# A fused attention and feed-forward kernel: the range check moves to GpSimd, the decayed state to VectorE

## What is computed

```python
for t in range(S):                       # attention, per batch and head
    cur = einsum('bhd,bhe->bhde', u * k_t, v_t)
    y[t] = einsum('bhd,bhde->bhe', r_t, state + cur)
    state = w_t[..., None] * state + einsum('bhd,bhe->bhde', k_t, v_t)
h = x @ w_in;  solu = h * softmax(h);  x = layernorm(solu, g_ln) @ w_out   # expert 1
h = x @ w_in2; x = maximum(0.01 * h, h) @ w_out2                           # expert 2
```

## Time and profile before

| | |
|---|---|
| median of three runs | 825.48 us (825.39 to 825.62) |
| profiled execution: its own time | 825.48 us |
| profiled execution: span | 823.7 us |
| TensorE matmul (PE) busy | 786.2 us, 95% |
| VectorE (DVE) busy | 521.3 us, 63% |
| ScalarE (ACT) busy | 338.8 us, 41% |
| GpSimd (POOL) busy | 196.7 us, 24% |
| mean granted TensorE clock | 0.978 |

### The profile page before, as it was taken

One profiled execution on the slowest core, in us unless ns is written; L12 is line 12 of the kernel. 1 busy time (PEld: TensorE's weight loads), 2 busy tenths in 40 slices (PEclk: granted clock), 3 DMA queues, 4 the chain that ended last, 5 costly groups with the idle time before them and its releaser, 6 DMA issues.

```text
span 823.7 us, 11957 instructions
## 1 busy us (share of the span) xinstructions
PE 786.2 (95%) x4570; PEld 746.2 (91%) x4570; DVE 521.3 (63%) x1068; ACT 338.8 (41%) x652; POOL 196.7 (24%) x216
## 2 busy tenths in 40 slices
PE   2877999999999999999999999999999999999996
PEld 2655999999999999999999999999999999999996
DVE  7778776576575676667665765666765775553332
ACT  3335644344433444434434444335443444334332
POOL 4477823113111221121221131122131121000000
PEclk9976899999999999999999999999999999999999
DMA  7772211203202302203202122113112030000000
GB/s 193 248 228 58 58 30 29 58 2 87 58 1 58 87 1 58 58 1 88 58 1 58 28 61 58 29 29 87 29 30 58 1 87 30 1 1 29 1 0 32
DMA packets 18847, 43.50 MB, mean 53 GB/s; under 512 B 2272, under 2 KB 14688, under 8 KB 18400
## 3 DMA queue, kind: packets, MB, share of 16 engines
q1 hardware_dynamic: 14736, 33.24, 16.5%
q10 hardware_dynamic: 4048, 9.44, 3.3%
HBM read 37.95 MB, written 4.72 MB: 52 GB/s over the span
## 4 chain that ended last, share of the span: by engine, by line
PE 85%; DVE 0%; ACT 0%; issue 0%; ACTq 0%
PE BANKS L964 60%; PE MISC L964 21%; PE BANKS L1075 2%; PE MISC L994 1%; PE MISC L987 1%; DVE Rraw L863 0%; DVE RL L869 0%; ACT RH L633 0%; ACT Rraw L626 0%; DVE X2L L875 0%; ACT X2H L638 0%; ACT OUT L644 0%; DVE A L745 0%; DVE nmean L817 0%; ACTq L248 0%
## 5 line engine op out<-in xcount | busy, mean ns | idle before, releaser
L626 ACT ACTIVATE Rraw<-BANKS 128x384 f32<-128x384 f32 x128 | 62.9, 492 | 239.5 <-PE BANKS L964 237.8
L863 DVE TENSOR_TENSOR Rraw<-BANKS,Rraw 128x384 f32<-128x384 f32 x128 | 71.3, 557 | 133.5 <-ACT Rraw L626 133.0
L964 PE MATMUL BANKS<-RH,W4H 128*128 128x384 f32 x384 | 138.6, 361 | 0.9 <-DVE RL L869 0.8
L964 PE MATMUL BANKS<-X2H,W3H 128*128 128x384 f32 x384 | 130.4, 339 | 0.2 <-DVE X2L L875 0.2
L964 PE MATMUL BANKS<-X2L,W3H 128*128 128x384 f32 x384 | 129.1, 336 | 0.0
L964 PE MATMUL BANKS<-RL,W4H 128*128 128x384 f32 x384 | 129.1, 336 | 0.0
L964 PE MATMUL BANKS<-X2H,W3L 128*128 128x384 f32 x384 | 129.0, 336 | 0.0
L964 PE MATMUL BANKS<-RH,W4L 128*128 128x384 f32 x384 | 129.0, 336 | 0.0
L633 ACT ACTIVATE RH<-Rraw 128x384 fp32r<-128x384 f32 x128 | 67.1, 524 | 73.2 <-DVE Rraw L863 73.2
L436 POOL TENSOR_TENSOR ke<-att 112x512 f32<-112x512 f32 x24 | 29.5, 1230 | 255.3 <-DVE att L739 255.3
L735 DVE RECIPROCAL ki<-att 112x128 f32<-112x128 f32 x96 | 90.1, 941 | 0.0
(11 more groups left out here) (117 smaller groups left out, 1509.3 us busy)
## 6 DMA issues: line engine op xcount, KB each, us to landing
att<-rkw SPq DMA_DIRECT2D x48, 288.0 KB, 4.9
rtok<-r_tok SPq DMA_DIRECT2D x24, 192.0 KB, 4.5
ktok<-k_tok SPq DMA_DIRECT2D x24, 192.0 KB, 4.6
vtok<-v_tok SPq DMA_DIRECT2D x24, 192.0 KB, 4.7
out<-OUT SPq DMA_DIRECT2D x8, 576.0 KB, 5.6
W3raw<-w_in ACTq DMA_DIRECT2D x1, 3072.0 KB, 11.2
W4raw<-w_out ACTq DMA_DIRECT2D x1, 3072.0 KB, 24.3
W1raw<-w_in ACTq DMA_DIRECT2D x1, 1536.0 KB, 9.5
```

The costliest lines, as they stand in the source:

```text
L626: nc.scalar.activation(Rraw[:, fp % 2, :], PR[fp % 2][:, 0:ST], ACT.Copy, scale=0.01).then_inc(act_slope, 1)
L863: nc.vector.tensor_tensor(Rraw[:, fp % 2, :], PR[fp % 2][:, 0:ST], Rraw[:, fp % 2, :], ALU.max).then_inc(dve_relu, 1)
L964: return nc.tensor.matmul(dst, lhsT, rhs, start=start, stop=stop, skip_group_check=True)
```

## The change

Three things change. The reciprocals are written into `ke` itself, so `ki` and `junk` go, and `inverse` waits for the transposes of the previous chunk's `ke` in place of the range sums. The range check becomes one sum: `end_keys` on GpSimd first adds `ke` (the reciprocals) and `ct` into a spare place (`range_of`: a part of `LN` for the first three chunks, `A` for the others), then makes the end keys, and ScalarE sums that place in one pass in slot 1 of the chunk. The mask of pair 0 waits for this pass where `A` is the place. And `decayed_state` goes from GpSimd: VectorE writes the masked new part into `fresh`, waits for it, and forms the state in four instructions, one per pair.

```diff
+        def range_of(b, m):
+            place = LN[:, CPS - 1, 0:PAIRS * CH] if first(b, m) else A[:, :, :, :].rearrange("p a h t -> p (a h t)")
+            return place[0:PD, :].rearrange("p (a t) -> p a t", a=PAIRS)
             def end_keys(b, m):
                 wait(pool, dve_keys, chunks(b, m, 1, 1))
-                wait(pool, pe_keT, chunks(b, m))
+                if first(b, m):
+                    wait(pool, act_range, m)
+                else:
+                    wait(pool, pe_y, chunks(b, m, PAIRS))
+                nc.gpsimd.tensor_tensor(range_of(b, m), ke[:, :, :], ct[:, p, :, :], ALU.add).then_inc(pool_range, 1)
+                wait(pool, pool_range, chunks(b, m, 1, 1))
                 nc.gpsimd.tensor_tensor(ke[:, :, :], kt[:, p, :, :], last, ALU.mult).then_inc(pool_ke, 1)
-            def decayed_state(b, m):
-                wait(pool, dve_state, states(b, m - 1))
-                nc.gpsimd.tensor_tensor(fresh[:, :, :], state[:, :, :], last, ALU.mult).then_inc(pool_decay, 1)
...
-                        if 0 < m % CPB < CPB - 1:
-                            decayed_state(b, m)
...
-            def take_range(b, m):
-                wait(act, dve_inv, chunks(b, m, PAIRS, PAIRS))
-                for i, part in enumerate((ki[:, :, :], ct[:, m % 2, :, :])):
-                    wait(act, act_range, chunks(b, m, 2, i))
-                    nc.scalar.activation(junk[:, :, :], part, ACT.Copy,
-                                         accum_out=spread[:, bass.ds(chunks(b, m, 2, i), 1)]).then_inc(act_range, 1)
...
             def item_end(b, m, s, attend=True):
-                if attend and s == 7 and exists(b, m) and exists(b, m + 1):
-                    take_range(b, m + 1)
+                if attend and s == 1 and exists(b, m):
+                    wait(act, pool_range, chunks(b, m, 1, 1))
+                    nc.scalar.activation(range_of(b, m), range_of(b, m), ACT.Copy,
+                                         accum_out=spread[:, bass.ds(at, 1)]).then_inc(act_range, 1)
...
             def inverse(b, m, a):
                 if a == 0:
-                    wait(dve, act_range, chunks(b, m, 2))
+                    wait(dve, pe_keT, chunks(b, m))
                 wait(dve, dve_decay, chunks(b, m, PAIRS, a + 1))
-                nc.vector.reciprocal(ki[:, a, :], ct[:, m % 2, a, :]).then_inc(dve_inv, 1)
+                nc.vector.reciprocal(ke[:, a, :], ct[:, m % 2, a, :]).then_inc(dve_inv, 1)
...
             def mask(b, m, a):
+                if a == 0 and not first(b, m):
+                    wait(dve, act_range, chunks(b, m, 1, 1))
...
             def take_state(b, m):
-                    wait(dve, pool_decay, fresh_count(b, m))
-                    for h in range(2):
-                        cols = slice(h * D, (h + 1) * D)
-                        ins = nc.vector.scalar_tensor_tensor(
-                            state[:, :, cols], own[:, :, cols], heads[:, h * D:h * D + 1], fresh[:, :, cols],
-                            ALU.mult, ALU.add)
+                    nc.vector.tensor_tensor(fresh[:, :, :], own, which, ALU.mult).then_inc(dve_fresh, 1)
+                    wait(dve, dve_fresh, fresh_count(b, m))
+                    for a in range(PAIRS):
+                        ins = nc.vector.scalar_tensor_tensor(
+                            state[:, a, :], state[:, a, :], ct[:, m % 2, a, CH - 1:CH], fresh[:, a, :],
+                            ALU.mult, ALU.add)
```

More of the change, by code:

```diff
@@ L134, in build @@
         ke = sb("ke", [PD, PAIRS, CH])
-        ki = sb("ki", [PD, PAIRS, CH])
-        junk = sb("junk", [PD, PAIRS, CH])
         rb = sb("rb", [PD, PAIRS, 2, CH])
@@ L162, in build @@
         mhalf = sb("mhalf", [CH, 1])
-        spread = sb("spread", [PD, 2 * NCH])
+        spread = sb("spread", [PD, NCH])
         total = sb("total", [PD, 1])
@@ L215, in build @@
         dve_decay, dve_inv, dve_keys, dve_masked = sem("dve_decay"), sem("dve_inv"), sem("dve_keys"), sem("dve_masked")
-        dve_diag, dve_y, dve_state = sem("dve_diag"), sem("dve_y"), sem("dve_state")
+        dve_diag, dve_y, dve_fresh, dve_state = sem("dve_diag"), sem("dve_y"), sem("dve_fresh"), sem("dve_state")
         dve_x, dve_max, dve_nmax, dve_he = sem("dve_x"), sem("dve_max"), sem("dve_nmax"), sem("dve_he")
@@ L221, in build @@
             sem("pool_q"), sem("pool_ke"), sem("pool_ruk"), sem("pool_dv"), sem("pool_rstd"), sem("pool_bias"))
-        act_range, pool_decay = sem("act_range"), sem("pool_decay")
+        pool_range, act_range = sem("pool_range"), sem("act_range")
         judged, pe_tame, guarded = sem("judged"), sem("pe_tame"), sem("guarded")
@@ L433, in end_keys @@
                 wait(pool, dve_keys, chunks(b, m, 1, 1))
-                wait(pool, pe_keT, chunks(b, m))
+                if first(b, m):
[4 more added lines that the diff above has]
+                wait(pool, pool_range, chunks(b, m, 1, 1))
                 last = ct[:, p, :, CH - 1:CH].broadcast_to([PD, PAIRS, CH])
                 nc.gpsimd.tensor_tensor(ke[:, :, :], kt[:, p, :, :], last, ALU.mult).then_inc(pool_ke, 1)
-            def decayed_state(b, m):
-                wait(pool, dve_state, states(b, m - 1))
-                last = ct[:, m % 2, :, CH - 1:CH].broadcast_to([PD, PAIRS, PC])
-                nc.gpsimd.tensor_tensor(fresh[:, :, :], state[:, :, :], last, ALU.mult).then_inc(pool_decay, 1)
             def own_token(b, m, part):
@@ L614, in item_end @@
             def item_end(b, m, s, attend=True):
-                if attend and s == 7 and exists(b, m) and exists(b, m + 1):
-                    take_range(b, m + 1)
+                if attend and s == 1 and exists(b, m):
+                    at = chunks(b, m)
+                    wait(act, pool_range, chunks(b, m, 1, 1))
+                    nc.scalar.activation(range_of(b, m), range_of(b, m), ACT.Copy,
+                                         accum_out=spread[:, bass.ds(at, 1)]).then_inc(act_range, 1)
                 for n in due(b, m, s, "rows"):
@@ L673, in _ @@
             part_heads(0, 0)
-            take_range(0, 0)
             for i in range(1, LEAD + 1):
@@ L732, in inverse @@
                 if a == 0:
-                    wait(dve, act_range, chunks(b, m, 2))
+                    wait(dve, pe_keT, chunks(b, m))
                 wait(dve, dve_decay, chunks(b, m, PAIRS, a + 1))
-                nc.vector.reciprocal(ki[:, a, :], ct[:, m % 2, a, :]).then_inc(dve_inv, 1)
+                nc.vector.reciprocal(ke[:, a, :], ct[:, m % 2, a, :]).then_inc(dve_inv, 1)
             def undecayed_keys(b, m):
                 wait(dve, dve_inv, chunks(b, m, PAIRS, PAIRS))
-                nc.vector.tensor_tensor(kt[:, m % 2, :, :], kt[:, m % 2, :, :], ki[:, :, :],
+                nc.vector.tensor_tensor(kt[:, m % 2, :, :], kt[:, m % 2, :, :], ke[:, :, :],
                                         ALU.mult).then_inc(dve_keys, 1)
@@ L915, in _ @@
             run(B - 1, batch_steps(True))
-            dve.wait_ge(act_range, 2 * NCH)
+            dve.wait_ge(act_range, NCH)
             nc.vector.tensor_reduce(total[:, :], spread[:, :], AX.X, ALU.add).then_inc(judged, 1)
```

## The result

The changed kernel takes 835.62 us (median of four, 833.29 to 835.84) against 825.55 of the kernel before (four, with one more than above): a ratio of 1.0113, 95% interval 1.0094 to 1.0133. It is slower, as forecast, but by 10.1 us and not by 2.3, and outside the range. The profiled execution took 836.03 us (span 834.3), against 825.48 (823.7).

What follows compares the result with a forecast made beforehand. TensorE was taken as the bound, full from 105 us on, with losses only in the start. (a) to (d) gave 2.0 us at 80 us; with (e), (f) and the clock, +2.3: 827.8 us, range 826.2 to 829.4.

Steps and rivals of the forecast that it cites:

- the steady part at 0: After the start: slack hides the later end keys and state, so 0 us, with 0 to 1 for the range.
- The price of the state update, +0.7 us: VectorE, each of 16 chunks: product and four short instructions cost 0.7 us more than the L771 pair (0.3 to 1.35).
- The work by engine: Whole kernel: ScalarE 19 us less work, VectorE 11 us more, GpSimd 10 to 14 us more.
- (a): Second chunk's scans, from 13.3 us: GpSimd's extra addition holds the fourth scan too, delaying mask and token loads by 0.8 us.
- (b): Third chunk's values and scans, to 57 us: 0.7 of the 0.8 us is carried there (0.3 to 0.9).
- (c): Third chunk, L781 at 66.72 us: the state before it is 0.7 us longer, so +0.2 (0 to 0.9).
- (d): Fourth chunk, from 69.3 us: GpSimd's addition goes in front of L436 in a chain without cover, +1.1 us.
- (e): Fourth chunk, L781 at 92.65 us: the longer state costs +0.6, or 0 if TensorE's clock makes it late.
- (f): Fifth chunk, L436 at 98.98 us: addition costs 1.0, GpSimd is 0.6 us earlier, so +0.4 (0 to 1.0).
- The clock, -1.0 to +0.9: Start: -1.0 us if the clock still rises at 90.5 us; rising with the work or later, 2.0 to 2.9 in all.
- one turn worse: Rival, 1%: a further 3 us at half clock cost 1.5 us, giving 829.3 us.
- the rivals: Delay absorbed in the start (27%, 826.4 us), VectorE binding the steady part (7%, 833), faster (5%, 823.7), clock worse (1%, 829.3).

Runs made afterwards that it cites:

- e3_state_psum: The changed kernel with the masked new part written back into its PSUM bank, so the four short instructions read one SBUF operand: 828.64 us.
- e2_range_only: The changed kernel with the state part undone (GpSimd decays the state again, two instructions L771); the new range check stays: 829.32 us.
- the fillers in the changed kernel: The changed kernel with unread 128x128 products on TensorE behind the transposes of y in the third and fourth chunk: 834.71 us.
- e6_add_behind: e3_state_psum with the reciprocals in a tile of their own again and GpSimd's range-check addition behind the end keys: 827.38 us.
- the kernel before with fillers: The kernel before with unread 128x512 products on TensorE ahead of the third and fourth chunk's first products with the values: 826.91 us.

## Why the prediction was wrong, point by point

**What bounds the kernel; the steady part at 0.** Right. TensorE is as full as before, its waits are 1.5 us, and the state part from the fifth chunk on measures as nothing.

**The price of the state update, +0.7 us.** Right where nothing holds it: in e3_state_psum the four take 0.99 us (0.85 assumed), with 0.56 for the product, so 1.6 against 0.74, +0.8. The estimate that the prediction worked out from the Trainium skill's "VectorE: DVE Perf Modes" (the section on the TRN2 errata) was 0.16 us for one short instruction. The trace doesn't agree: it has 0.31, and 0.25 for each of four in a row.

**The work by engine.** ScalarE has 18.8 us less over the whole span (19 forecast), VectorE 16.7 more (11) and GpSimd 18.9 more (10 to 14). GpSimd's surplus comes from the additions, 1.5 us each on average where 1.05 to 1.23 was taken, and some 5.5 us of VectorE's is the hold of the state update.

**(a) +0.8.** The mechanism was right, with the size somewhat off: 1.3 us at the scans (4.57 for 3.28). The new addition takes 1.26 us and not 1.05, and GpSimd starts its run 0.35 us later (13.64 for 13.29), because the first scan does. An addition there alone is +0.9 at the end, with the reserve said above.

**(b) 0.7 carried to the third chunk.** 1.5 us. It is the 1.4 us of (a) at the mask (18.38 for 17.01) carried on, of which 0.35 was already there at the first scan (8.19 after, 7.84 before), which waits for its load.

**(c) +0.2 for the state ahead of `XL` in the third chunk.** This step failed. It took the 0.7 us of an undisturbed update minus 0.42 of slack, and put the hold by GpSimd's split at nothing. Product and four instructions take 3.4 us where L771 took 0.74. TensorE lost 2.4 us from 57 to 71 us, and the chunk alone costs 3.3 at the end.

**(d) +1.1.** Right, with 1.3 measured: from the end of GpSimd's one-column instruction to that of `ke` it is 80.12 - 77.51 = 2.6 us, against 74.92 - 73.64 = 1.3. Moving the addition behind gives 1.3 us back in this chain, and 0.9 at the end, which the intervals neither confirm nor exclude.

**(e) 0 to +0.6 in the fourth chunk.** This failed for the same reason, and it is the largest miss: 4.0 us between the transposes of y and the first product with W1, and 5.4 at the end for the chunk alone.

**(f) +0.4.** Not seen in the changed kernel: with TensorE so late, `ke` of the fifth chunk (from 104.33 on) is there long before it is wanted (110.51). The key product did come through sooner, as the step says (1.16 us in place of 3.13). In e2_range_only, where TensorE is earlier, it was held for 6.87, and TensorE did wait for `ke`.

**The clock, -1.0 to +0.9.** The low clock lasted longer, 44 us of the start for 34, as in the rival "one turn worse". TensorE loses 2.1 us between the fourth chunk's first product with W1 and the fifth chunk's transposes, where its products run at half clock to 107 us (0.63 us each for 512 columns, 0.40 after). What the clock costs by itself stays open: the fillers in the changed kernel met a longer hold.

What was missing in (c) and (e) was in the prediction's own rows. Step (a) read from the earlier trace rows that a scan, with both operands in SBUF, waits for GpSimd's instruction to end. The diff gives the state update the same kind of operands, and puts it beside splits of 2.35 us. The key product of the kernel before (3.13 us for 0.68 at 92.56) is a plainer row of the same kind, and wasn't used. I priced it by the size of its data and by L771, which reads PSUM. The Trainium skill has the rule in "SBUF — State Buffer", in the section on SBUF's two separate sides: VectorE with two SBUF inputs and a GpSimd instruction that reads SBUF share a pair of ports, and whichever starts first keeps it for its whole instruction. The trace agrees with it three times: 2.13 and 2.42 us behind splits of 2.35, 1.15 us for a scan behind one of GpSimd's products of about 1 us, and 0.99 for four once an operand comes from PSUM.

None of the rivals named it either: they put the cost into the steady part, the clock or nowhere.

No version here beats the kernel before. The nearest with both parts of the change is e6_add_behind, at +1.2 us.

## What to carry to other kernels

Before an operand is moved from PSUM to SBUF, list which GpSimd instructions can run at that moment, and price the VectorE instruction at no less than the longest of them, with everything queued behind it. Look at every stage of the kernel: the same edit cost nothing in 13 chunks, where no instruction was held, and some 7 us in the start, nearly all of it in two. Where the data come from PSUM anyway, try writing the intermediate back in place there: here the hold was gone with the same number of instructions.

## What the runs showed of the hardware that was not expected

A 112x96 instruction with two tensor operands and a scalar takes 305 to 321 ns with its second tensor in SBUF, where it isn't held, and 305 to 316 ns with it in PSUM.

Who goes next between GpSimd and VectorE wasn't the same everywhere. A GpSimd instruction of one column lasted 4.35 us beside three VectorE splits run back to back (3.49 us), in both kernels. GpSimd's own runs let a scan or a 112x96 instruction through after each instruction (1.15 us a scan in the earlier trace rows, one of the four behind each split in the fourth chunk). But the 112x512 key product of e2_range_only, started at 93.76, came to its end only behind the last of four splits, at 100.6, though by their mean length of 2.37 us two of the earlier ones ended in between. What decides it, no run here shows.

Half clock on TensorE can be nearly free where it waits anyway: the kernel before with fillers has 27 us of it in the start in place of 34, and the same time.
